# Picking one expert's rows in a TensorE loop over staged tiles, and one layer moved ahead of the transposes

## The chip, the core and the metric

The kernel runs on one core of a Trainium2 chip. A core has TensorE (matrix products, with its weight loads recorded apart), VectorE, ScalarE and GpSimd for the rest, and SyncE, which here only issues DMAs. One on-chip memory (SBUF) feeds all of them, and TensorE's results land in the eight banks of another (PSUM). The engines run side by side and wait for each other by counters (semaphores). The metric is the device time of one execution in microseconds (us), as the median of several.

## What is computed

Sparse attention over 4 batches x 8 heads x 576 positions, then a mixture of eight experts over the 2304 tokens, then one more feed-forward layer over all tokens. The change lies between the first and the second. This is the mixture:

```python
skip_score = x @ w_skip                  # x: 2304 tokens x 512
xc = x[skip_score > 0]
logits = xc @ w_gate                     # 8 experts
e_idx = argmax(logits); gate_w = softmax(logits)[e_idx]
for e in range(8):
    mask = e_idx == e
    h = relu(xc[mask] @ w1[e])           # 512 x 1024
    y[mask] = gate_w[mask] * (h @ w2[e]) # 1024 x 512
out[do_compute] = xc + y
```

## The kernel before, in words

The attention leaves x transposed in `XT` (512 rows of x as 4 blocks of 128 partitions, 2304 columns). The tokens must then be sorted by expert. The steps in order:

- TensorE turns each of the 18 tiles of 128 tokens back into rows (L967), ScalarE copies them into `xrow` (L572, counter `rows_copied`). VectorE meanwhile works out the expert and the place of every token and, for each tile t, a mask `hot(t)` of 128 x 168 that says which token goes to which of the first 168 sorted places (L736, counter `hot_ready`).
- GpSimd scatters each tile's rows to their sorted place in DRAM, `x_sorted` (L469, 18 indirect DMAs, counter `scattered`).
- TensorE doesn't wait for that round trip. It picks the first expert's 168 rows itself: for each of the four column blocks c it sums over the 18 tiles `xrow[:, t, c]` times `hot(t)` into bank `first_b[c]` (L995, unrolled; one float32 matmul of the code is two MATMUL and two LDWEIGHTS records, so 144 products). Each finished c raises `first_picked`; VectorE copies c = 0 and 2 (L765), ScalarE c = 1 and 3 (L580).
- `into(0)`: first layer of expert 0 (L1031, 64 products), ScalarE's `relus` (L588) behind it.
- `second_rows()`: the 168 rows of the second expert, loaded from `x_sorted` (SyncE L380 and L381, once `scattered` is full), are transposed (L1002) and copied by VectorE and ScalarE (L767, L592).
- `sort_turned()`: all sorted rows come back from DRAM into `xrow` by six loads (SyncE L385, which wait for `first_picked` to be 4, since they overwrite `xrow`), are transposed tile by tile (L1014, 72 transposes; L1018 for the gates) and copied into `XT` by VectorE (even tiles, L777) and ScalarE (odd tiles, L596), through the four banks `bank[2:6]`.
- `into(1)`, then `outof(0)`: second layer of expert 0 (L1041), whose results go to the same four banks. From expert 2 on, `into(e)` and `outof(e-1)` alternate.

Two side chains matter. The gates go through DRAM: VectorE copies them (L781), SyncE stores them (L396) and waits, and GpSimd, once they are stored and all of `XT` is sorted, copies the window of expert 2 (L476), which `into(2)` waits for. And SyncE issues its DMAs in the order of the code: the second expert's rows, the six loads, `w2` of expert 1 (L386), two small ones, then `w1` of expert 2 after `into(0)`.

Counters of TensorE's own products, such as `first_picked`, are raised when the product is done. All code of TensorE is unrolled here, apart from a loop over the attention's middle steps (L938), which runs three times, and one over the later groups of the last layer.

Of the kernel before, what the change touches and what calls it, by code (L numbers as in the profile page):

```python
# [9 lines left out]
F32 = mybir.dt.float32  # L10
# [8 lines left out]
P = 128  # L19
# [5 lines left out]
NT = N // P  # L25
# [88 lines left out]
def program(nc, qT, kT, vl, vs, wg, w1, w2, win, wout, cst, out):  # L114
    with ExitStack() as ctx:
        def sem(name):
            return ctx.enter_context(nc.semaphore(name))
# [37 lines left out]
        gateT, _, o = at("gateT", [GATES * E, NT // GATES, P], F32, p_at)  # L155
        gates, _, o = at("gates", [P, NT // GATES, GATES * E], F32, o)
        assert o <= r_end

# [97 lines left out]
        scattered, pads_out = sem("scattered"), sem("pads_out")  # L256
        gates_flat = sem("gates_flat")
        slots_in, hot_ready, first_picked, first_copied = sem("slots_in"), sem("hot_ready"), sem("first_picked"), sem("first_copied")
        second_in, second_turned, second_copied = sem("second_in"), sem("second_turned"), sem("second_copied")
# [24 lines left out]
        def hot(t):  # L284

            return XT[:, t % DC, WIN * (t // DC):WIN * (t // DC + 1)]
# [14 lines left out]
        def _(sp):  # L301
# [80 lines left out]

            sp.wait_ge(first_picked, DC)
            for g in range(NS):
# [148 lines left out]
        def _(act):  # L533
# [36 lines left out]
            for t in range(NT):  # L570
                act.wait_ge(rows_ready, t + 1)
                act.copy(xrow[:, t, 0:D], row_b[t % 4][:, :]).then_inc(rows_copied, 1)  # L572
                if t == EXP_AT:
                    act.wait_ge(dif_ready, 1)
                    act.activation(ex[:, :, :], dif[:, :, :], ACT.Exp).then_inc(exp_ready, 1)

            act.wait_ge(more_ready, 1)
            for c in range(1, DC, 2):
                act.wait_ge(first_picked, c + 1)
                act.copy(xw[:, 0, c, :], first_b[c][:, 0:WIN]).then_inc(first_copied, 1)  # L580
# [10 lines left out]
            act.wait_ge(second_turned, 2)  # L591
            act.copy(xw[:, 1, :, P:WIN], second_b[1][:, 0:DC * (WIN - P)].rearrange("p (c n) -> p c n", c=DC)).then_inc(second_copied, 1)  # L592

            for t in range(1, NT, 2):
                act.wait_ge(xt_ready, t + 1)
                act.copy(XT[:, :, P * t:P * (t + 1)], sort_b[t % 4][:, :].rearrange("p (c n) -> p c n", c=DC)).then_inc(xt_act, 1)  # L596
            more_n = act.value_load(n_more[0:1, 0:1], min_val=0, max_val=EXTRA)
            for e in range(1, E):
                relus(e, e % 2)
# [52 lines left out]
        def _(dve):  # L652
# [108 lines left out]


            for c in range(0, DC, 2):
                dve.wait_ge(first_picked, c + 1)
                dve.tensor_copy(xw[:, 0, c, :], first_b[c][:, 0:WIN]).then_inc(first_copied, 1)  # L765
# [85 lines left out]
        def _(pe):  # L851
# [137 lines left out]

            for c in range(DC):  # L990
                for t in range(NT):
                    if c == 0:
                        pe.wait_ge(rows_copied, t + 1)
                        pe.wait_ge(hot_ready, t + 1)
                    last = pe.matmul(first_b[c][:, 0:WIN], xrow[:, t, P * c:P * (c + 1)], hot(t), start=(t == 0), stop=(t == NT - 1))  # L995
                last.then_inc(first_picked, 1)

# [36 lines left out]
            def outof(e, par, loads):  # L1034
                pe.wait_ge(w2_in[par], 16 * loads)
                for c in range(DC):
                    behind(pe, y_scaled, DC * (e - 1) + c + 1)
                    for f in range(FEC):
                        if c == 0:
                            pe.wait_ge(h_done, FEC * e + f + 1)  # L1040
                        last = pe.matmul(y_b[c][:, 0:WIN], WE2[:, par, f, P * c:P * (c + 1)], hid[:, par, f, :], start=(f == 0), stop=(f == FEC - 1))  # L1041
                    last.then_inc(y_ready, 1)

            into(0, 0, 0, 1)
            second_rows()
            sort_turned()
            into(1, 1, 1, 1)

            pe.wait_ge(xt_dve, NT // 2)
            pe.wait_ge(xt_act, NT // 2)  # L1050
            outof(0, 0, 1)
# [139 lines left out]
```

## Time and profile before

| | us |
|---|---|
| median of 3 runs | 687.55 (687.15 to 689.2) |
| profiled execution | 690.49 |
| its span, first to last instruction | 688.4 |
| TensorE busy in it | 655.7 (95%) |
| picking (L995), first start to last end | 92.19 to 128.4 |

The span is the time between the first and the last instruction of one profiled execution; 2.1 us lie around it. Times inside it are counted from its start. Engines are named in the rows as PE (TensorE), PEld (its weight loads), DVE (VectorE), ACT (ScalarE), POOL (GpSimd) and SPq (SyncE's queue of DMA issues). A busy time says nothing by itself: an engine that waits for nobody and for whom nobody waits costs nothing. The chain of waits is what sets the end.

### The profile page before, as it was taken

Reading aid. Unit: us, or ns where it says so; the run is one execution under the profiler, and the core shown is the slowest. Engines: PE = TensorE matmul, PEld = TensorE weight load, DVE = VectorE, ACT = ScalarE, POOL = GpSimd, SP = SyncE. Lnnn points to the kernel's source line nnn. Section 1 sums busy time; section 2 is a strip of 40 time slices with the busy share of each in tenths; the row PEclk is TensorE's granted clock in tenths of the full one; section 3 lists DMA queues with packets and bytes.
Section 4 is the critical chain, followed back from the end, with each engine's and each line's share of the span. In section 5 each row is a group of like instructions: output and inputs, shape, how many; then the busy total and the mean of one; then the engine's idle time right before and its main releaser. Section 6 shows DMA issues by size and latency. Waiting matters only on the chain.

```text
span 688.4 us, 12667 instructions
## 1 busy us (share of the span) xinstructions
PE 655.7 (95%) x5265; PEld 567.6 (82%) x5266; DVE 317.6 (46%) x588; ACT 187.8 (27%) x361; POOL 126.1 (18%) x134
## 2 busy tenths in 40 slices
PE   7888995999999999999999999999999999999995
PEld 3776694999999999878888888888888888888994
DVE  4767460042121121676456544456444565545652
ACT  2455440141111111132224222232222332223331
POOL 1333155003222224882000200002000020000201
PEclk9999995999999999999999999999999999999999
DMA  8686595495777775230000100001000010000100
GB/s 279 207 282 206 181 388 186 172 357 160 259 256 261 263 274 189 85 115 17 0 1 1 61 1 0 1 0 61 0 0 0 0 61 0 0 0 1 62 0 31
DMA packets 39469, 76.09 MB, mean 111 GB/s; under 512 B 2967, under 2 KB 18012, under 8 KB 38916
## 3 DMA queue, kind: packets, MB, share of 16 engines
q1 hardware_dynamic: 36548, 66.00, 28.1%
q0 software_dynamic: 2880, 9.52, 3.6%
q8 instruction: 29, 0.48, 0.3%
q14 instruction: 12, 0.10, 0.0%
HBM read 65.57 MB, written 9.94 MB: 110 GB/s over the span
## 4 chain that ended last, share of the span: by engine, by line
PE 90%; DMA 4%; DVE 2%; issue 2%; SPq 1%; POOL 1%; ACT 0%; DVEq 0%
PE pair L1077 28%; PE pair L1096 16%; PE bank L1096 13%; PE pair L1031 11%; PE out_pair L1041 5%; PE bank L1041 5%; DMA k_loc<-kT 2%; PE pair L995 2%; PE out_pair L920 2%; PE pair L878 2%; PE out_pair L995 2%; DMA k_str<-kT 1%; PE bank L898 1%; PE bank L1014 1%; DVE yl L812 1%
## 5 line engine op out<-in xcount | busy, mean ns | idle before, releaser
L1077 PE MATMUL pair<-yh,WIH 128*128 128x512 f32 (+1 forms) x316 | 114.2, 368 | 0.2 <-ACT yh L609 0.2
L1077 PE MATMUL pair<-yh,WIL 128*128 128x512 f32 (+1 forms) x316 | 114.1, 368 | 0.0
L633 ACT ACTIVATE cl<-cl,half 128x512 f32<-128x512 f32 (+1 forms) x80 | 54.4, 680 | 185.1 <-DVE cl L833 183.7
L841 DVE TENSOR_TENSOR gl<-gr,gh 128x512 fp32r<-128x512 f32 (+1 forms) x80 | 54.5, 681 | 73.2 <-ACT gh L642 72.0
L833 DVE TENSOR_SCALAR cl<-pair 128x512 f32<-128x512 f32 (+1 forms) x79 | 50.3, 636 | 71.0 <-PE pair L1077 70.9
L528 POOL DMA_INDIRECT out<-XT,tok x18 | 18.6, 1031 | 349.4 <-DVE XT L821 345.4
L1077 PE MATMUL pair<-yl,WIH 128*128 128x512 f32 (+1 forms) x316 | 77.8, 368 | 0.4 <-DVE yl L812 0.4
L1031 PE MATMUL pair<-xw,WE 128*128 128x168 f32 x512 | 74.3, 306 | 0.5 <-ACT xw L580 0.5
L1031 PEld LDWEIGHTS pair<-xw,WE 128*128 128x128 f32 x512 | 73.3, 190 | 0.7 <-issue 0.7
L642 ACT CAST gh<-gr 128x512 fp32r<-128x512 f32 (+1 forms) x80 | 46.3, 579 | 85.6 <-PE bank L1096 58.3
L1077 PEld LDWEIGHTS pair<-yh,WIH 128*128 128x128 f32 x316 | 59.5, 188 | 11.0 <-ACT yh L609 0.6
L1077 PEld LDWEIGHTS pair<-yh,WIL 128*128 128x128 f32 x316 | 59.5, 188 | 10.3
L1077 PEld LDWEIGHTS pair<-yl,WIH 128*128 128x128 f32 x316 | 56.0, 189 | 10.6 <-DVE yl L812 0.8
L1096 PE MATMUL pair<-WOH,gh 128*128 128x512 f32 x160 | 62.6, 391 | 1.0 <-DVE gl L841 0.9
L839 DVE TENSOR_TENSOR gr<-gr,cl 128x512 f32<-128x512 f32 (+1 forms) x80 | 53.1, 664 | 21.9 <-ACT cl L633 21.6
L1096 PE MATMUL pair<-WOL,gh 128*128 128x512 f32 x160 | 62.4, 390 | 0.0
L1096 PE MATMUL pair<-WOH,gl 128*128 128x512 f32 x160 | 62.1, 389 | 0.0
L1096 PE MATMUL bank<-WOH,gh 128*128 128x512 f32 x128 | 49.8, 389 | 0.0
L1096 PE MATMUL bank<-WOL,gh 128*128 128x512 f32 x128 | 49.8, 389 | 0.0
L1096 PE MATMUL bank<-WOH,gl 128*128 128x512 f32 x128 | 49.8, 389 | 0.0
L836 DVE TENSOR_SCALAR gr<-pair 128x512 f32<-128x512 f32 (+1 forms) x79 | 49.5, 627 | 0.0
L588 ACT ACTIVATE hid<-pair 128x168 f32<-128x168 f32 x64 | 19.9, 311 | 108.3 <-PE pair L1031 108.3
(154 smaller groups left out, 849.6 us busy)
## 6 DMA issues: line engine op xcount, KB each, us to landing
WE<-w SPq DMA_DIRECT2D x16, 2048.0 KB, 10.9
xrow<-x_sorted SPq DMA_DIRECT2D x6, 781.5 KB, 9.8
v_loc<-vl SPq DMA_DIRECT2D x4, 1024.0 KB, 6.7
raw_in<-win SPq DMA_DIRECT2D x16, 256.0 KB, 9.2
raw_out<-wout SPq DMA_DIRECT2D x16, 256.0 KB, 2.6
q_loc<-qT SPq DMA_DIRECT2D x4, 576.0 KB, 5.3
k_loc<-kT SPq DMA_DIRECT2D x4, 576.0 KB, 6.9
v_str<-vs SPq DMA_DIRECT2D x8, 256.0 KB, 4.4
```

The costliest lines, as they stand in the source:

```text
L588: act.activation(hid[:, par, f, :], hid_b[f % 2][:, 0:WIN], ACT.Relu).then_inc(h_done, 1)
L633: act.activation(cl[:, 0:n], cl[:, 0:n], ACT.Square, bias=half[:, :], scale=0.5).then_inc(squared, 1)
L642: act.copy(gh[:, f % 2, 0:n], gr[:, 0:n]).then_inc(g_high, 1)
L833: dve.tensor_scalar(cl[:, 0:n], h2_of(g, f)[:, 0:n], -1.0, 1.0, ALU.max, ALU.min).then_inc(clamped, 1)
L836: dve.tensor_scalar(gr[:, 0:n], h2_of(g, f)[:, 0:n], 1.0, -1.0, ALU.max, ALU.add).then_inc(over, 1)
L839: dve.tensor_tensor(gr[:, 0:n], gr[:, 0:n], cl[:, 0:n], ALU.add).then_inc(g_ready, 1)
L841: dve.tensor_tensor(gl[:, f % 2, 0:n], gr[:, 0:n], gh[:, f % 2, 0:n].bitcast(F32), ALU.subtract).then_inc(g_low, 1)
L995: last = pe.matmul(first_b[c][:, 0:WIN], xrow[:, t, P * c:P * (c + 1)], hot(t), start=(t == 0), stop=(t == NT - 1))
L1031: last = pe.matmul(hid_b[f % 2][:, 0:WIN], WE1[:, par, c, P * f:P * (f + 1)], xw[:, buf, c, :], start=(c == 0), stop=(c == DC - 1))
L1041: last = pe.matmul(y_b[c][:, 0:WIN], WE2[:, par, f, P * c:P * (c + 1)], hid[:, par, f, :], start=(f == 0), stop=(f == FEC - 1))
L1077: last = pe.matmul(h2_of(g, f)[:, 0:tokens], w[:, c, P * f:P * (f + 1)], x[:, c, 0:tokens], start=(not low and c == 0 and k == 0), stop=(l ...
L1096: last = pe.matmul(fin_b[t][:, :], x[:, f % 2, P * t:P * (t + 1)], w[:, f, :], start=(f == 0 and k == 0), stop=(f == FFC - 1 and k == 2))
```

## The change

The picking now runs tile by tile: for each tile the four column blocks are multiplied one after the other into the four banks, which stay open over all tiles. Tile 0 and tile 17 are read from `xrow` as before. Tiles 1 to 16 are read from a new ring `stage` of four tiles, which ScalarE fills by copies from `xrow` after its last row copy, so that a TensorE loop of four passes over four tiles has fixed addresses for its weights. Two counters link the two: `staged` and `tile_picked`. `first_picked` is raised once, at the end. `into(1)` moves ahead of `sort_turned()` on TensorE, its `relus(1, 1)` ahead of the copies on ScalarE, and `outof(0)` waits for VectorE's copies ahead of its first and for ScalarE's ahead of its second column block.

```diff
+        stage, _, o = at("stage", [P, DC, D], F32, o)
...
-            sp.wait_ge(first_picked, DC)
+            sp.wait_ge(first_picked, 1)
...
+            for t in range(1, NT - 1):
+                behind(act, tile_picked, t - DC)
+                act.wait_ge(rows_copied, t + 1)
+                act.copy(stage[:, t % DC, :], xrow[:, t, 0:D]).then_inc(staged, 1)
+
             act.wait_ge(more_ready, 1)
+            act.wait_ge(first_picked, 1)
             for c in range(1, DC, 2):
-                act.wait_ge(first_picked, c + 1)
                 act.copy(xw[:, 0, c, :], first_b[c][:, 0:WIN]).then_inc(first_copied, 1)
...
+            relus(1, 1)
             for t in range(1, NT, 2):
                 act.wait_ge(xt_ready, t + 1)
...
-            for e in range(1, E):
+            for e in range(2, E):
                 relus(e, e % 2)
...
+            dve.wait_ge(first_picked, 1)
             for c in range(0, DC, 2):
-                dve.wait_ge(first_picked, c + 1)
...
-            for c in range(DC):
-                for t in range(NT):
-                    if c == 0:
-                        pe.wait_ge(rows_copied, t + 1)
-                        pe.wait_ge(hot_ready, t + 1)
-                    last = pe.matmul(first_b[c][:, 0:WIN], xrow[:, t, P * c:P * (c + 1)], hot(t), start=(t == 0), stop=(t == NT - 1))
-                last.then_inc(first_picked, 1)
+            def pick(rows_of_tile, table, first, last):
+                for c in range(DC):
+                    picked = pe.matmul(first_b[c][:, 0:WIN], rows_of_tile[:, P * c:P * (c + 1)], table, start=first, stop=last)
+                return picked
+
+            pe.wait_ge(rows_copied, 1)
+            pe.wait_ge(hot_ready, 1)
+            pick(xrow[:, 0, :], hot(0), True, False)
+            assert (NT - 2) % DC == 0
+            with pe.Fori(0, (NT - 2) // DC) as i:
+                for t in range(1, DC + 1):
+                    pe.wait_ge(staged, DC * i + t)
+                    pe.wait_ge(hot_ready, DC * i + t + 1)
+                    pick(stage[:, t % DC, :], XT[:, t % DC, bass.ds(WIN * i + WIN * (t // DC), WIN)], False, False).then_inc(tile_picked, 1)
+            pe.wait_ge(rows_copied, NT)
+            pe.wait_ge(hot_ready, NT)
+            pick(xrow[:, NT - 1, :], hot(NT - 1), False, True).then_inc(first_picked, 1)
...
                 for c in range(DC):
+                    if isinstance(e, int) and e == 0 and c < 2:
+
+                        pe.wait_ge(xt_act if c else xt_dve, NT // 2)
...
             into(0, 0, 0, 1)
             second_rows()
+            into(1, 1, 1, 1)
             sort_turned()
-            into(1, 1, 1, 1)
-
-            pe.wait_ge(xt_dve, NT // 2)
-            pe.wait_ge(xt_act, NT // 2)
             outof(0, 0, 1)
```

## Rows read from the trace of the kernel before

**Rows 1.** The page: TensorE's busy time, its 40 slices and its clock.

```profile
PE 655.7 (95%) x5265; PEld 567.6 (82%) x5266; DVE 317.6 (46%) x588; ACT 187.8 (27%) x361; POOL 126.1 (18%) x134
PE   7888995999999999999999999999999999999995
PEclk9999995999999999999999999999999999999999
```

**Rows 2.** Chain that ended last, in order of time: start us, us, what.

```profile
92.35 9.23 PE out_pair L995 x63
101.59 0.41 issue
...
106.23 0.28 PE pair L995
...
114.52 1.66 issue
...
117.62 10.78 PE pair L995 x58
...
128.86 9.36 PE pair L1031 x64
138.22 0.45 PE bank L1002 x4
...
147.74 9.12 PE pair L1031 x64
156.86 4.56 PE bank L1041 x32
...
165.98 9.12 PE pair L1031 x64
```

**Rows 3.** Busy us (and count) in stretches; clock, DMA share, GB/s; first three: L995 alone.

```profile
92.20:101.30 9.10, 9.10 (x63) 8.92 (x63) 1.00 1.03 396
102.00:117.60 15.60, 7.75 (x23) 5.36 (x23) 0.60 0.56 213
117.60:128.40 10.80, 10.77 (x58) 10.51 (x58) 0.79 0.11 32
...
120.00:124.00 4.00, 4.00 (x22) 4.00 (x22) 0.33 (x1) 0.00 (x0) 0.00 (x0) 0.72 0.00 0
...
136.00:140.00 4.00, 3.58 (x29) 3.30 (x28) 0.69 (x1) 1.20 (x4) 0.00 (x0) 1.00 1.05 391
```

**Rows 4.** DMA queues (packets, MB, share of 16), 98 to 100 us, then 102 to 117.

```profile
q0 software_dynamic: 136, 0.45, 57.1%
q1 hardware_dynamic: 94, 0.34, 41.5%
q8 instruction: 1, 0.02, 2.9%
...
q0 software_dynamic: 1004, 3.32, 57.8%
```

**Rows 5.** GpSimd's scatters; SyncE's issues (start us, us); what SyncE waited for.

```profile
L469 POOL DMA_INDIRECT x_sorted<-xrow,slot_of x18: 957/963/1142, 91.9 to 113.7; - x18
...
116.87 0.70 SPq L380 DMA_DIRECT2D xsecond<-x_sorted  x1
...
128.41 4.70 SPq L385 DMA_DIRECT2D xrow<-x_sorted  x6
...
SPq L385 <- PE pair L995: 10.4, 1, 10.4
```

**Rows 6.** Timeline of three engines: start us, us, what, [idle before <- releaser].

```profile
92.19 9.40 PE L995 MATMUL out_pair<-XT,xrow 128*128 128x168 f32 x63
...
90.80 4.01 DVE L736 TENSOR_SCALAR XT<-slots,posf 128x168 f32<-128x168 f32 x18
...
102.72 0.33 DVE L765 COPY xw<-out_pair 128x168 f32<-128x168 f32 x1 [4.58 <-remote]
...
92.28 1.25 ACT L572 COPY xrow<-pair 128x512 f32<-128x512 f32 x2
117.84 0.30 ACT L580 COPY xw<-out_pair 128x168 f32<-128x168 f32 x1 [24.31 <-remote]
```

**Rows 7.** The attention: chain at 34 to 37 us, TensorE's waits, queues 40 to 74.

```profile
34.64 0.37 PE bank L898 x2
35.01 1.82 issue
36.83 0.37 PE bank L898
...
PE bank L898 <- issue: 1.8, 1, 1.8
...
q1 hardware_dynamic: 4652, 8.11, 73.1%
q14 instruction: 2, 0.02, 0.1%
```

**Rows 8.** Output scatter: GpSimd's issues, and all engines' busy us in stretches.

```profile
552.65 0.96 POOL L528 DMA_INDIRECT out<-XT,tok  x1 [81.57 <-DVE XT L821]
...
552.00:556.00 4.00, 4.00 (x19) 3.30 (x18) 3.02 (x5) 0.81 (x3) 2.74 (x3) 1.00 0.32 122
556.00:560.00 4.00, 4.00 (x20) 3.30 (x19) 2.58 (x4) 1.81 (x3) 1.10 (x2) 1.00 0.37 140
```

**Rows 9.** ScalarE's copies, grouped: busy us, mean ns, idle before.

```profile
L642 ACT CAST gh<-gr 128x512 fp32r<-128x512 f32 (+1 forms) x80 | 46.3, 579 | 85.6 <-PE bank L1096 58.3 <-DVE gr L839 27.3
...
L572 ACT COPY xrow<-pair 128x512 f32<-128x512 f32 x10 | 5.9, 671 | 3.5 <-PE pair L967 3.5
```

**Rows 10.** Timeline around the end of the transposes: VectorE, TensorE, GpSimd.

```profile
139.44 1.09 PE L1014 MATMUL bank<-con,xrow 128*128 128x128 f32 x8 [0.42 <-DVE xw L767]
...
147.23 0.69 DVE L777 COPY XT<-bank 128x512 f32<-128x512 f32 x1
...
147.57 9.29 PE L1031 MATMUL pair<-xw,WE 128*128 128x168 f32 x64
...
155.24 0.74 POOL L476 COPY xw<-XT 128x672 f32 x1 [40.61 <-issue]
```

More of the change, by code:

```diff
@@ L257, in program @@
         gates_flat = sem("gates_flat")
+        staged, tile_picked = sem("staged"), sem("tile_picked")
         slots_in, hot_ready, first_picked, first_copied = sem("slots_in"), sem("hot_ready"), sem("first_picked"), sem("first_copied")
```

## The prediction

> **What bounds the kernel now.** I read five views, in this order: the page, the chain of waits in order of time, the idle time of TensorE's lines, the busy time by stretch, and the queues. The page says that TensorE is busy for 95% of the span, and that in the slices between 103 and 120 us its granted clock is half [rows 1]. So a gain has to come out of a place where TensorE stands still or runs at half clock. The chain has one such place, the picking of the first expert's rows (L995). Its 144 products start at 92.19 us [rows 6] and the last ends at 128.40 us [rows 2]. The first 63 start one every 0.144 us (9.10 us for 63). The next 23 take 15.6 us, and between them the chain shows "issue", which is time that no wait of the profile explains. The last 58 take 10.8 us, 0.186 us each [rows 2, 3]. At the pace of the first 63, all 144 would take 144 x 0.144 = 20.8 us. They take 36.2 us, so 15.4 us are lost: some 12.3 us in the 23 slow ones and some 2.4 us in the last 58, which start at the lower clock (0.79 in the mean of that stretch; the two levels are 1.2 and 2.4 GHz, and the fall comes after TensorE had stood still repeatedly). Behind the picking the chain is TensorE alone: the first layer of expert 0, the second expert's window, 72 transposes, the first layer of expert 1, the second layer of expert 0 [rows 2].
>
> What the stall is, is the whole question. Three things happen around it. One block of code (q8) is fetched between 98 and 100 us. GpSimd's 18 scatters of the rows run from 91.9 to 114.6 us, and their packets alone fill the queues from 102 to 117 us. SyncE, which waits for the scatters, goes on at 116.87 us, 0.75 us before TensorE is fluent again [rows 4, 5]. And the two engines that wait for TensorE's counter get it late: the first column block is finished at some 97.5 us, VectorE's copy of it starts at 102.72; the second at 106.2, ScalarE's copy starts at 117.84 [rows 2, 6].
>
> **The loop over staged tiles.** Two readings of the stall give two results. In the first, TensorE is short of code: a straight run of 144 products needs 288 instructions to be brought in while the queues are full, and a loop whose body is brought in once doesn't. For it: the attention's loop body runs three times, its only "issue" wait of TensorE (1.82 us) comes once, in the first pass, and in 34 us of the later passes the queues carry no packet of q8 [rows 7], whose packets of 16 KB come where TensorE's straight code goes on. Also for it: while the output is scattered by the same kind of DMA, four tiles at a time, TensorE stays busy 4.00 of 4 us [rows 8]. In the second reading the scatter itself slows whatever TensorE sends and receives. For that: the late counters above, and an end that falls on the scatter's end. I take the first, with little more than an even chance.
>
> The new picking then goes like this. Tile 0 is multiplied at once: 8 products x 0.144 = 1.16 us, to 93.35 us. ScalarE has its last row copy behind it at 93.53 us [rows 6]. It then copies tile 1 to the stage. That copy has no row of its own; the nearest are 579 ns (128x512 within the on-chip memory, L642) and 671 ns (the row copies L572, whose starts are 0.48 us apart) [rows 9]. I take 0.58 us: staged at 94.1 us, so TensorE waits 0.75 us. From there it needs 8 x 0.144 = 1.16 us for a tile and ScalarE at most 0.68 us, so ScalarE stays ahead, as long as the counter tile_picked, which frees a stage four tiles later, arrives in time (a rival, below). 17 tiles x 1.16 = 19.7 us, so the last product ends at about 114.0 us. The masks are no limit: VectorE has all 18 at 94.8 us [rows 6]. What the loop adds is two waits, a register or two and three jumps back. No row prices them; they lie in the queue ahead of the array, so between nothing and 1.8 us for each jump (the 1.82 us of [rows 7]); I take 0.5 us in all.
>
> The picks now end together, where before three of four columns were copied behind the next. So two copies on each engine stand on the path instead of one: +0.33 us [rows 6]. The first layer of expert 0 starts at 114.0 + 0.33 + 0.33 + 0.14 = 114.8 us instead of 128.86: 14.0 us earlier. What ScalarE gained to do (16 copies, 9.3 us) lies in 24.3 us in which it was idle [rows 6]. If that cover were gone, TensorE would wait for each tile.
>
> **What comes due next.** SyncE's order puts the second expert's window (L380) ahead of the sorted rows, and that waits for the scatters, to 116.87 us, whatever the picking does. Its own wait for the picking (10.4 us) goes [rows 5]. So the six loads of the sorted rows start at about 118 instead of 128.41 us. They are 4.7 MB and at the 390 GB/s of the stretch behind them [rows 3] take some 12 us, to 130 or 131 us. With the old order TensorE would want the first of them at 114.8 + 9.2 + 1.4 = 125.4 and the last some 7 us later, so they would cost up to 2 us there. With the first layer of expert 1 put before (9.1 us), the transposes start at 134.7 us and everything has landed. This is what the second part buys: not 9 us, but cover for 0 to 2 us. The window itself has landed by 120 us, when the queues are empty [rows 3], and is wanted at 124.
>
> **The second part by itself** moves 64 products ahead of 72 transposes on TensorE, and 8 activations ahead of 9 copies on ScalarE. VectorE's order stays. The wait for the window's copy (0.42 us, [rows 10]) only moves. The second layer of expert 0 now stands right behind the transposes and needs their last copies: VectorE's ends at 147.92 where TensorE is through at 147.57 [rows 10], so +0.4 us, which the first layer of expert 1 used to cover. GpSimd's window for expert 2 waits for all copies and for the gates' way through memory: 147.9 to 155.24, 7.3 us, with a weight load in the queues [rows 10]. It is wanted when the second layer of expert 0 ends: before the change at 165.98 us [rows 2], 18.3 us behind the transposes, after it 0.4 + 9.1 = 9.5 us behind them, with 7.3 + 0.74 us to go. It is hidden, but by 1.5 us only; if the gates came 2 us later it would show. I put it at nothing, because w1 of expert 2 follows the sorted rows in SyncE's order, and should be through by then.
>
> **Sum.** -14.0 + 0.4 + 0.5 = -13.1 us. The profiled execution took 690.49 us (span 688.4 and 2.1 around it), the median of the runs shown is 687.55, 2.9 us less. So 690.49 - 13.1 = 677.4 for a profiled execution and 674.5 us for the median, 1.9% less. All times below are medians.
>
> **Rivals.**
> (a) The loop pays for its jumps. If each of the three jumps back costs what the one code stall of the attention cost, 1.82 us [rows 7], 5.5 us of the gain go: 674.5 + 5.5 = 680 us. The Trainium skill has a rule that speaks for this (Runtime: NRT & Kernel Launch, Instruction fetch mechanics): prefetch is sequential, a taken branch whose target lies outside the buffered window must fetch first, hence its advice to unroll. The same section gives TensorE room for 2048 instructions. The passes without a fetched block in [rows 7] agree with the second sentence and speak against (a).
> (b) The stall belongs to the scatter, not to the code. Then TensorE is as far behind at 117.6 us as now, less 5 products for the 0.75 us wait: 63 instead of 58 are left, +0.9 us, and +0.33 and +0.4 us of the above. Nothing is gained: 687.55 + 1.6 = 689.2 us, within the measurement. For it: the late counters and the end of the stall. Against: [rows 8] and the single stall of [rows 7]. This is also the case in which the change doesn't do what it says.
> (c) Slower: the stage's ring closes on a late counter. A stage is free again when tile_picked reaches ScalarE, and between 97.5 and 117.6 us TensorE's counter was 5.2 and 11.6 us late [rows 2, 6]. The ring covers four tiles less a copy, 4 x 1.16 - 0.58 = 4.1 us. It decides from a lateness over 4.1 us. With 11.6 us, four tiles take 12.2 us: from tile 3 at 97.5 us it gets to tile 10 by 117.6 us, and with more instructions per tile in a throttled queue perhaps only to tile 6. Left are then 7 to 11 tiles x 8 x 0.186 = 10 to 16 us, against 10.8 now. With the 0.7 us above this is +0.5 to +6; I take +4: 691.5 us.
>
> **How the numbers follow.** Forecast 0.50 (its own range 673 to 678), (a) 0.07, (b) 0.23, (c) 0.20. A measurement of this kernel tells apart about 0.3%, 2 us, from no change. Faster by more than that: 0.57. Within: 0.22, which is (b) nearly whole. Slower: 0.21, which is (c) and the end of (b). Cases of both signs hold most of the chance, so the range reaches from the forecast's lower end to (b) and the first half of (c): 673 to 691.
>
> **What would show it.** In the changed kernel's profile: TensorE's "issue" between 98 and 118 us gone, and no half clock there; the last picking product at 114 us; ScalarE's stage copies 1.16 us apart after the fourth; the six sorted loads at 118 us; a wait of some 0.4 us ahead of the second layer of expert 0, and none for GpSimd's window behind it. For (b): "issue" gaps of the same kind inside the loop, ending near 117.6 us. For (c): TensorE waiting for ScalarE's stage copies, and these for TensorE, in rounds of four. For (a): a gap at every fourth tile. The prediction is wrong if TensorE is not through tile 12 by 110 us.

## The result, and the profile after

The changed kernel takes 691.3 us (median of 12), the kernel before beside it 687.4: a ratio of 1.0053 (95% interval 1.0031 to 1.0074), so 0.5% slower, where the prediction forecast 674.5 us in a range of 673 to 691. The profiled execution took 692.06 us (span 690.0), 1.6 us more than that of before.

The page of after, the lines that answer to [rows 1]. TensorE is busy for 2.6 us less than before in a span that is 1.6 us longer, so it stands idle for 4.2 us more, and the half clock stands in the same slice:

```profile
PE 653.1 (95%) x5266; PEld 566.0 (82%) x5266; DVE 318.3 (46%) x588; ACT 197.1 (29%) x377; POOL 125.9 (18%) x134
PEclk9999995999999999999999999999999999999999
```

The chain of waits of after, in order of time (start us, us, what), beside [rows 2]. The picking is L1001 now. "Another core or an unknown queue", and "remote" in the timelines, is a wait whose source the trace doesn't tell:

```profile
99.11 0.57 PE out_pair L1001 x4
99.68 1.08 PE pair L1001 x4
...
100.81 3.54 issue
104.35 0.02 ACT stage L583
104.37 9.07 another core or an unknown queue
...
113.49 2.86 another core or an unknown queue
...
116.38 0.63 ACT stage L583
...
117.23 1.48 PE out_pair L1001 x4
...
127.94 0.58 PE pair L1001 x4
128.52 0.02 issue
128.55 0.58 DVE xw L774 x2
...
129.26 9.36 PE pair L1050 x64
...
157.61 4.80 PE bank L1063 x32
```

Up to 100 us the loop runs as forecast, a tile every 1.14 us. Then 17 us pass in which the chain goes through ScalarE's stage copies and through something that it can't name. The first layer of expert 0 starts at 129.26 us, where it started at 128.86 [rows 2]. The picking itself began 1.14 us earlier than before (91.05 against 92.19 us), so from its first product on this is 1.5 us more.

The timeline of after, ScalarE and then TensorE (start us, us, what, [idle before <- releaser]):

```profile
92.09 2.33 ACT L583 COPY stage<-xrow 128x512 f32<-128x512 f32 x4
94.59 0.62 ACT L583 COPY stage<-xrow 128x512 f32<-128x512 f32 x1 [0.17 <-PE pair L1001]
96.52 0.62 ACT L583 COPY stage<-xrow 128x512 f32<-128x512 f32 x1 [1.31 <-PE pair L1001]
100.79 0.62 ACT L583 COPY stage<-xrow 128x512 f32<-128x512 f32 x1 [3.65 <-PE pair L1001]
104.35 0.62 ACT L583 COPY stage<-xrow 128x512 f32<-128x512 f32 x1 [2.95 <-issue]
113.47 0.62 ACT L583 COPY stage<-xrow 128x512 f32<-128x512 f32 x1 [8.50 <-remote]
116.38 2.18 ACT L583 COPY stage<-xrow 128x512 f32<-128x512 f32 x4 [2.29 <-remote]
...
101.64 0.83 PE L1001 MATMUL out_pair<-XT,stage 128*128 x4 [1.39 <-issue]
...
105.20 1.48 PE L1001 MATMUL out_pair<-XT,stage 128*128 x4 [2.16 <-issue]
...
114.34 1.48 PE L1001 MATMUL out_pair<-XT,stage 128*128 x4 [6.54 <-issue]
```

The copies of tiles 7, 8 and 9 start at 100.79, 104.35 and 113.47 us; TensorE takes these tiles up 0.85 to 0.87 us after each start. So TensorE waits for the stage (though two of its gaps are put down to "issue"), and ScalarE waits for `tile_picked`. Tile 9 may be copied when tile 5 is picked. TensorE was through with it at about 99 us, by the pace of 1.14 us a tile; the copy starts 14 us later. Tile 10 needs tile 6, which was picked at 100.25 us, and is copied at 116.38, 16 us later. The ring covers some 4 us of lateness. That is the wait that rival (c) names.

SyncE in after, beside [rows 5]. The loads of the sorted rows start where they did, since the picking ends where it did:

```profile
115.58 0.67 SPq L382 DMA_DIRECT2D xsecond<-x_sorted  x1
...
128.54 4.51 SPq L387 DMA_DIRECT2D xrow<-x_sorted  x6
```

### The profile page after: what moved, and what is told of

The parts are those of the page before. It is cut to its first block, busy times and chain, and to the rows that moved or that the text cites. A ratio compares the mean times of both kernels' runs of the same rounds, so it can differ in the third digit from the quotient of the medians.

```text
span 690.0 us, 12724 instructions
## 1 busy us (share of the span) xinstructions
PE 653.1 (95%) x5266; PEld 566.0 (82%) x5266; DVE 318.3 (46%) x588; ACT 197.1 (29%) x377; POOL 125.9 (18%) x134
## 4 chain that ended last, share of the span: by engine, by line
PE 85%; DMA 6%; DVE 2%; another core or an unknown queue 2%; ACT 2%; issue 1%; POOL 1%; SPq 1%; DVEq 0%
PE pair L1096 27%; PE pair L1115 16%; PE bank L1115 13%; PE pair L1050 10%; PE bank L1063 5%; PE out_pair L1063 5%; DMA k_loc<-kT 2%; DMA WE<-w 2%; PE out_pair L929 2%; PE pair L887 2%; PE out_pair L1001 1%; PE pair L1001 1%; ACT xrow L574 1%; DMA k_str<-kT 1%
## 5 line engine op out<-in xcount | busy, mean ns | idle before, releaser
L848 DVE TENSOR_TENSOR gr<-gr,cl 128x512 f32<-128x512 f32 (+1 forms) x80 | 53.0, 663 | 21.8 <-ACT cl L642 21.8
```

The source lines that it names most:

```text
L848: dve.tensor_tensor(gr[:, 0:n], gr[:, 0:n], cl[:, 0:n], ALU.add).then_inc(g_ready, 1)
```

## The experiments

The runs were made on five chips, here A to E. The kernel before took, as a median on each: A 688.7, B 676.7, C 689.2, D 676.6, E 690.1 us. That turned out to matter more than any edit. Every ratio is to the kernel before on the same chip. Each chip was used at one time only, so these runs can't tell the chip from the time.

**The scatter moved behind the picking (chip A).** Is the scatter the source? In both kernels GpSimd waits for the picking (for 1 instead of DC in the changed one):

```diff
+            pool.wait_ge(first_picked, DC)
             for t in range(NT):
                 pool.wait_ge(rows_copied, t + 1)
```

> The kernel before with one wait added: GpSimd begins its 18 scatters only when the picking is through (first_picked at 8). Nothing is left out. Scatter theory (the scatter delays what TensorE sends and receives): the picking takes 20.8 us (92.2 to 113.0 us), without 'issue' in the chain, at full clock, and both copies of the first two column blocks start within 0.1 us of their last product. Code theory (TensorE is short of instructions while queues are full): the queues are empty here too, so the picking is fluent as well, but with the counters of the column blocks as late as before only if something else delays them; so this run alone tells little between the two, and says only that the scatter is or isn't the source. If the stall belongs to neither (for example to the length of the straight code), it stays, at 98 to 118 us. The price: the scatters then run from 113 to about 136, SyncE's loads of the second window and the sorted rows behind them; the transposes, which ended at 147.6 us, end about 5 to 8 us later. Ratio to before expected 1.007 to 1.012. If the stall exists only in profiled executions, the timed runs would be worse by some 19 us instead (1.028).

> The changed kernel with the same wait: GpSimd begins its scatters when the picking is through (first_picked at 1). Nothing is left out. With the scatter out of the way the loop stands alone: if tile_picked is late only because of the scatter, the stage copies follow each other by 1.16 us, TensorE never waits for ScalarE over 0.1 us after the first tile, the picking takes 20.8 us plus 0.75 us (first stage) plus at most 0.5 us for the loop: 22 us, ending at 114.2 us. If the loop itself is slow (jumps back, a ring that is too short in any case), it takes 25 us or more, with gaps at every fourth tile. Against the kernel before with the same wait: the same or up to 1.5 us slower from the loop, and the second expert's first layer (9.36 us) now covers part of the wait for the sorted rows, so in the whole some 6 to 9 us faster than it; ratio to the kernel before 0.995 to 1.003.

Measured: 1.0168 (1.0125 to 1.0210) and 1.0132 (1.0083 to 1.0181). Timelines of the first (TensorE, ScalarE), then of the second (ScalarE):

```profile
88.91 10.43 PE L996 MATMUL out_pair<-XT,xrow 128*128 128x168 f32 x72
99.17 10.42 PE L996 MATMUL pair<-XT,xrow 128*128 128x168 f32 x72
...
99.42 0.30 ACT L581 COPY xw<-out_pair 128x168 f32<-128x168 f32 x1 [9.18 <-PE out_pair L996]
119.14 0.31 ACT L589 ACTIVATE hid<-pair 128x168 f32<-128x168 f32 x1 [1.64 <-PE pair L1032]
122.00 0.31 ACT L589 ACTIVATE hid<-pair 128x168 f32<-128x168 f32 x1 [2.55 <-remote]
```

```profile
94.06 0.62 ACT L584 COPY stage<-xrow 128x512 f32<-128x512 f32 x1 [0.52 <-PE pair L1002]
95.20 0.62 ACT L584 COPY stage<-xrow 128x512 f32<-128x512 f32 x1 [0.52 <-PE pair L1002]
```

Without the scatter beside it the unrolled picking has no gap (20.7 us), its counters are in time, and the ring never closes: the stage copies are 1.14 us apart. From the first product to the last, start to start, the loop takes 21.4 us and the unrolled form 20.4. The hold-up has moved with the scatters, which run from 110.62 us: of ScalarE's activations, 1.14 us apart until 117.19, the last two come 0.8 and 2.5 us late (119.14 and 122.00), while TensorE's products are fluent to their end at 119.43. So the scatter is needed for the stall, and the loop costs 1.1 us where nothing disturbs it. The price of the later scatter was underestimated in both (11.6 us instead of 5 to 8, and 9.1 instead of at most 2): the second expert's rows come late, and TensorE stands still for 18.9 us ahead of them in the trace of scatter_after.

**The two parts, one at a time.** `loop_only` is the first part alone. `layer_only` is the second alone, this swap with its waits and ScalarE's order:

```diff
-            sort_turned()
-            into(1, 1, 1, 1)
+            into(1, 1, 1, 1)
+            sort_turned()
```

> The changed kernel with the old order behind the picking: the sorted rows' transposes ahead of the first layer of expert 1, and both waits for the copies ahead of the second layer of expert 0. Nothing is left out. If the loop's ring alone makes the change slower, the whole difference is here: ratio 1.003 to 1.007, and the second layer of expert 0 starts as late as in the changed kernel or up to 0.5 us earlier. If the order costs too (copies of the last tiles, ScalarE's 8 activations ahead of its copies), this run is at 1.000 to 1.003.

> The kernel before with the second part of the change alone: the first layer of expert 1 ahead of the sorted rows' transposes, its activations ahead of ScalarE's last copies, the second layer of expert 0 waiting for the copies. Nothing is left out. By the forecast the order alone costs 0.4 us (the copies of the last tiles stand on the path); the sorted rows are loaded in time in either order. Ratio 1.000 to 1.001. If the order is what makes the change slower, 1.002 or more, and a new wait shows behind the transposes or at the gates.

Measured: the loop alone on A 1.0038 (1.0010 to 1.0067). The order alone on B 0.9953 (0.9932 to 0.9974). The second was a surprise, and its trace a greater one. TensorE and GpSimd on chip B:

```profile
91.68 10.43 PE L996 MATMUL out_pair<-XT,xrow 128*128 128x168 f32 x72
101.94 10.42 PE L996 MATMUL pair<-XT,xrow 128*128 128x168 f32 x72
...
91.39 1.14 POOL L469 DMA_INDIRECT x_sorted<-xrow,slot_of  x1 [17.22 <-ACT xrow L572]
...
113.15 0.96 POOL L469 DMA_INDIRECT x_sorted<-xrow,slot_of  x1 [0.30 <-issue]
```

The scatters run as in [rows 5], 18 of them over the same 22 us, the code of the picking is that of before, and there is no stall at all.

**The chip or the code?** The kernel before, the changed kernel and the second part were run again on other chips:

> The kernel before, unchanged, for its trace on this chip. The run of layer_only had a picking without any stall, while its text up to the end of the picking is that of the kernel before, and the kernel before took 676.7 us beside it, 12 us less than in the earlier call. If the stall belongs to the chip, the trace goes with the time: at some 688 us with 'issue' between 101 and 117 us and 36 us of picking, at some 677 us without, and 20.5 us of picking. If it belongs to the text of the kernel (layer_only shifts it), the stall is here at either time.

> The changed kernel, unchanged, timed on this chip. Where TensorE has no stall, the counter tile_picked is in time, ring and loop cost 0.75 us for the first stage, 0.33 us for the second copy and at most 0.5 us for the loop, and the order of the first layer of expert 1 gives back what it gave in layer_only (0.47% or 3.2 us with its interval from 0.26 to 0.68%): ratio 0.995 to 1.000. Where TensorE has the stall, as before: 1.003 to 1.007, with stage copies that follow late counters. A ratio over 1.002 without the stall would mean that the loop costs by itself.

> The kernel before with the first layer of expert 1 ahead of the transposes, once more. Nothing is left out. If the stall is absent on this chip, the ratio is 0.993 to 0.998 as before, since the sorted rows are loaded from 115 us on and the old order would want them at 123. If the stall is there, the sorted rows come late in either order (their loads start when the picking ends, and have 10 us to land): 0.999 to 1.002.

> The changed kernel once more, for the case that this chip has no stall, where it hasn't been timed yet: then the picking takes 21.5 to 22.5 us, the stage copies follow each other by 1.14 us, and the ratio is 0.995 to 1.000 (the order of the first layer of expert 1 gives 0.3 to 0.6%, the loop takes up to 0.2%). With the stall it is 1.003 to 1.007 again.

> The changed kernel with the old order behind the picking, once more. Nothing is left out. Without the stall: the changed kernel was at 0.9998 and the order of the first layer alone at 0.9953, so the loop should cost 0.2 to 0.6% by itself (of which the first stage and the second copy explain 1.1 us, 0.16%): 1.002 to 1.006. If the order and the loop don't add up so (the order gives nothing behind a shorter way), 1.000 to 1.001. With the stall: 1.001 to 1.007 as before.

| | chips with the stall | chips without it |
|---|---|---|
| kernel before, us | A 688.7, C 689.2, E 690.1 | B 676.7, D 676.6 |
| picking, first to last product, unrolled | 34.2 to 35.9 us (4 traces, without small_ops2) | 20.4 us (B) |
| the same, in the loop | 36.8 to 39.2 us (4 traces) | 21.4 us (D) |
| changed kernel | first measurement 1.0053, C 1.0053 (1.0022 to 1.0084) | D 0.9998 (0.9981 to 1.0015) |
| loop alone | A 1.0038, E 1.0035 (1.0010 to 1.0061) | not run |
| order alone | C 0.9990 (0.9959 to 1.0021) | B 0.9953 (0.9932 to 0.9974) |

The second and third lines are starts of the first and last picking product in the timelines. The stall goes with the chip, not with the code: `layer_again` on C is the kernel of `layer_only` on B, and has a stall of 15 us. The 12 us between the chips' medians fit the stall, less what it hides, but there is no trace of the kernel before itself on B, D or E; on D its executions spread from 675.2 to 685.3 us, so a stall in some of them isn't excluded. On a chip without it the changed kernel does what the prediction describes, in its timings too, and gains nothing. Chain of the changed kernel on chip D:

```profile
91.40 0.83 PE out_pair L1001 x4
...
110.47 0.58 PE pair L1001 x4
...
111.80 9.36 PE pair L1050 x64
...
122.42 9.36 PE pair L1050 x64
```

No gap stands at any of the loop's jumps back.

**Aligned rows (chip A).** `ROW` of 528 instead of 521 numbers:

> The kernel before with rows of 528 instead of 521 numbers in the row tile and in its copy in memory (2112 bytes, a multiple of 64, instead of 2084), the seven further columns set to zero. Nothing is left out. If the scatter stalls TensorE because its rows of 2084 bytes are cut at uneven places, the stall shrinks: the picking ends before 125 us instead of 128.4, ratio under 0.995. If it is the software-issued transfers as such, nothing changes: stall from 101 to 117 us, ratio 0.998 to 1.002.

Measured 0.9979 (0.9958 to 0.9999). The picking ends at 127.1 us, not before 125, with its stall from some 102 to 117.5 us. So the alignment isn't the cause; the ratio lies just under the 0.998 that was expected for this, and a gain of up to 0.4% from it isn't excluded.

**GpSimd's transfers or their bytes?** The 18 scatters become 18 plain stores by SyncE, the same tiles to the same buffer; the sorting is left out.

```diff
-                pool.indirect_dma_start(xs, bass.IndirectOffsetOnAxis(slot_of[:, t:t + 1], 0), xrow[:, t, :], None).then_inc(scattered, 16)
+                sp.dma_start(xs[P * t:P * (t + 1)], xrow[:, t, :]).then_inc(scattered, 16)
```

> The kernel before with the 18 scatters by GpSimd replaced by 18 plain stores of the same row tiles by SyncE, in the order of the tokens, to the same place in memory. The sorting of the rows is left out, so the experts get other rows; everything else stays. If the stall comes from transfers whose addresses GpSimd issues, it is gone: the picking takes 20.8 to 22 us and ends at about 113 to 114 us, with both first counters in time. If it comes from the bytes (3.8 MB out of the row tiles while TensorE reads them), the stall stays, some 10 to 15 us, wherever the stores run.

> As plain_store2, for a chip on which the kernel before takes some 688 us (the sorting of the rows is left out, the same rows go to memory in the order of the tokens by plain stores of SyncE). Stall from GpSimd's transfers: none here, picking 20.5 us. Stall from the bytes or the row tiles: 'issue' in the picking while the stores run. Where the kernel before takes some 677 us it tells nothing new.

Two runs fell on B and D and say nothing (674.2 and 671.6 us, picking fluent). The third fell on E, where the kernel before takes 690 us: 673.8 us. TensorE's timeline there:

```profile
91.36 10.43 PE L996 MATMUL out_pair<-XT,xrow 128*128 128x168 f32 x72
101.62 10.42 PE L996 MATMUL pair<-XT,xrow 128*128 128x168 f32 x72
...
129.44 1.09 PE L1015 MATMUL bank<-con,xrow 128*128 128x128 f32 x8 [0.57 <-DMA xrow<-x_sorted]
```

The queues are fuller than with the scatter (a DMA share of 1.06 from 102 to 110 us, against 0.56 in before_again), the bytes are the same, and there is no stall. So neither the bytes nor the reading of the row tiles is enough: it takes the scatters that GpSimd issues. Two things differ at once here, who issues the transfers and whether each row has an address of its own. Which of the two matters was not tested.

**Who is held up (chip C)?** VectorE and ScalarE get 150 and 60 copies of two columns, which need nothing and signal nothing:

```diff
+            for k in range(150):
+                dve.tensor_copy(tiny[:, k, :], con[:, C_ID:C_ID + 2])
```

> The kernel before with 150 copies of two columns on VectorE and 60 on ScalarE added ahead of their waits for the picking, so that both engines work while the scatter runs. Nothing is left out. If TensorE has its stall on this chip, two cases: the scatter holds up every engine that has many short instructions, and their starts spread between 101 and 117 us; or it holds up TensorE alone, and the copies follow each other at an even pace right through (60 to 200 ns each). Without the stall the run only says that the copies cost nothing.

Measured 690.4 us in one execution. VectorE's timeline, then the busy time by stretches (us, then PE, PEld, DVE, ACT, POOL with their counts, clock, DMA share, GB/s) of this kernel and of the kernel before on the same chip:

```profile
97.25 1.79 DVE L765 COPY tiny<-con 128x2 f32<-128x2 f32 x23
...
107.18 0.17 DVE L765 COPY tiny<-con 128x2 f32<-128x2 f32 x1 [1.22 <-issue]
107.89 0.17 DVE L765 COPY tiny<-con 128x2 f32<-128x2 f32 x1 [0.55 <-issue]
108.59 0.17 DVE L765 COPY tiny<-con 128x2 f32<-128x2 f32 x1 [0.53 <-issue]
...
116.29 7.28 DVE L765 COPY tiny<-con 128x2 f32<-128x2 f32 x103 [0.54 <-issue]
```

```profile
101.00:116.00 15.00, 3.89 (x10) 2.31 (x9) 3.19 (x20) 3.11 (x19) 9.60 (x10) 0.56 0.57 218
```

```profile
92.00:98.00 6.00, 6.00 (x44) 6.00 (x43) 4.26 (x19) 0.15 (x1) 4.78 (x5) 1.00 1.03 408
101.00:116.00 15.00, 7.05 (x24) 5.00 (x23) 0.00 (x0) 0.00 (x0) 9.47 (x10) 0.65 0.54 209
```

The copies come 0.08 us apart until 99 us, then one to three every 0.7 or 1.4 us, then again 0.07 us apart. TensorE, VectorE and ScalarE are held up together, and they share what is left: TensorE's two kinds of instructions fall from 47 to 19 in these 15 us, and VectorE and ScalarE get 39; together 58 against 47, where 107 were recorded in 6 us before the stall. GpSimd isn't held up: 18 scatters start over 21.8 us with the stall and without it (before, layer_only). It isn't TensorE's instruction supply, since copies on two other engines are held up at the same time, and it isn't signals alone, since these copies raise no counter. Nor is code fetched at any rate that would fit a start every 0.7 us. The queue of code from 92 to 117 us in before_again:

```profile
q8 instruction: 1, 0.02, 0.2%
```

**Does it take a run of scatters?** `layer_only`, with GpSimd waiting ahead of its seventh scatter:

```diff
+                if t == 6:
+                    pool.wait_ge(first_picked, DC // 2)
```

> layer_only with GpSimd's scatters in two parts: the first six at once, the other twelve when half of the picking is done (first_picked at 4/2, at some 102 us). Nothing is left out. On a chip with the stall it began some 8 to 9 us after the first scatter in every trace, about seven scatters later. If it needs such a run of scatters, it now begins at 110 us or later and TensorE has all but the last 15 instructions of the picking behind it: the picking ends before 116 us, and what stalls is the first layer of expert 0, until the scatters end at some 120 us; ratio 0.990 to 0.997. If it needs only some number of scatters since the start, it begins after the first one or two of the second part, ends at 120 us instead of 117, ratio 1.000 to 1.005. Without the stall: the second window lands 2.5 us later, ratio 0.995 to 1.000.

> layer_only with the first six scatters at once and the other twelve behind the picking (first_picked at 4). Nothing is left out. On a chip with the stall: the picking has none and ends at 113 us; the scatters end at 128.5, the second expert's rows are there at 132, TensorE waits for them from 122.5 us; the sorted rows land by 144, the transposes end at 150 to 152 instead of 156.9 us: ratio 0.991 to 0.996. If six scatters are enough to start the stall, it shows from 101 to some 103 us and the gain is 1 to 2 us less. Without the stall it is worse than layer_only by some 10 us: ratio 1.008 to 1.012.

> As split_mid (first six scatters at once, twelve behind half of the picking, the first layer of expert 1 ahead of the transposes), for a chip with the stall: if the stall needs a run of some seven scatters, TensorE is fluent to 109 us or later and the ratio is 0.990 to 0.997; if it counts scatters since the start, it begins at 103 to 104 us and the ratio is 1.000 to 1.005. Without the stall, 0.994 to 0.999 again.

Measured: split_mid on D 0.9965 (0.9936 to 0.9994), on E 0.9917 (0.9882 to 0.9951), where the stall is. split_end on D 1.0160 (1.0143 to 1.0177), some 3 us above the upper end of what was expected: in its trace the chain runs through the twelve later scatters and the second expert's load, and TensorE gets to that window only at 135.6 us. Timelines of split_mid2 on E: GpSimd, TensorE, ScalarE, VectorE:

```profile
96.94 0.96 POOL L471 DMA_INDIRECT x_sorted<-xrow,slot_of  x1 [0.30 <-issue]
101.44 0.96 POOL L471 DMA_INDIRECT x_sorted<-xrow,slot_of  x1 [3.54 <-PE out_pair L998]
...
101.00 10.42 PE L998 MATMUL pair<-XT,xrow 128*128 128x168 f32 x72
119.14 11.35 PE L1034 MATMUL pair<-xw,WE 128*128 128x168 f32 x64 [7.71 <-ACT xw L582]
...
118.70 0.30 ACT L582 COPY xw<-pair 128x168 f32<-128x168 f32 x1 [17.14 <-remote]
...
99.13 0.33 DVE L768 COPY xw<-out_pair 128x168 f32<-128x168 f32 x1 [2.53 <-remote]
```

The picking has no gap to its end at 111.4 us, though six scatters have run before 98 us and eight more by 111. Two of its four counters are late. The last product ends at 111.43, and ScalarE's copy starts at 118.70. And the first six scatters aren't without effect: the first column block ends at 95.94 us, and VectorE, idle for 2.53 us, copies it at 99.13, 3.2 us later. The first layer of expert 0 starts at 119.14, against 125.7 (C) and 128.9 us [rows 2]. So a pause of 3.5 us puts TensorE's first gap off by 10 us (111.4 against 101.3 us in before_again on C, whose picking starts at 90.8 us, as here at 90.6). The pause wasn't run without the second part.

**Wider products (chip B).** The mask as the weight and rows of 512 columns moving, 36 products instead of 72:

> The kernel before with the operands of the picking exchanged: the mask is the weight (40 or 128 slots), the row tile of 512 columns is what moves, so 36 products of 512 columns instead of 144 of 168; then 8 transposes bring the picked rows into the old layout. Nothing is left out. At 0.144 us for 168 columns a product of 512 should take 0.44 us, 36 of them 15.8 us. If the scatter holds up TensorE by instruction (some 0.7 us for a load and a product, whatever their size), the 36 products hardly feel it: the last ends at about 108 to 110 us, but its counter reaches VectorE only when the scatter is through (some 117 us), and the first layer of expert 0 begins at about 120 instead of 128.9 us: 8 to 9 us earlier, ratio 0.986 to 0.990. If it holds TensorE up by time (it stands still for 15 us, whatever it has to do), the last product ends at about 123 to 125 us, the first layer begins at 126 to 128, ratio 0.995 to 1.000.

Measured 1.0138 (1.0112 to 1.0164). My expectation priced a product by one record; it has two, as the text above says of those of 168 columns. They took 72 x 0.434 = 31.2 us instead of 20.5, which is more than the loss of 9.3 us. On this chip there was no stall to be seen through, so the question that it was made for stayed open there.

## Why the prediction was wrong

**What the stall is** is the step that failed: the reading that TensorE is short of code there, so that a loop ends the stall, and with it the term of -14.0 us. Measured, the first layer of expert 0 started 0.4 us later, not 14.0 us earlier. I took the code reading "with little more than an even chance". It is refuted: with the same code and the same scatters there is no stall on B; with GpSimd's transfers replaced there is none on E; and on C VectorE and ScalarE stall as well. What the runs showed in its place is a hold-up that comes with GpSimd's run of scatters and makes counters up to 16 us late. What I took for evidence was none:
- [rows 8] was put against the scatter, since TensorE stays busy in the output scatter. Those are four transfers at a time. In split_mid2 six in a row make one counter 3.2 us late and stop no product; TensorE's first gap in the unrolled picking came 9 to 11 us after the first of an unbroken run. A load that comes in small portions says nothing of a long run.
- [rows 7] and the block of q8 showed that code can stall TensorE once, not that it did here.
- The late counters were the right sign, and they stood in the rows: a shortage of code on TensorE doesn't explain the lateness of a counter whose product is done. They also came first: the first column block was finished at 97.48 us, 4 us before TensorE's first gap.

**Rival (c)** is what happened, with 0.20 as its chance: a ring of 4 us against counters that were 4 us late at tile 7 and 14 at tile 9. It forecast tile 10 at 117.6 us (117.23 in the trace) and 691.5 us (691.3 measured). The wait is the one that it names; that its numbers fit is luck in part. It had four tiles take 12.2 us from 97.5 us on; in the trace the pace was full to tile 6, and tiles 7 to 9 then took 17 us. And its +4 us was 3.3 us for the ring, where the picking took 1.3 us longer in the two traces of the result (37.16 against 35.89 us), and 0.7 us for copies. With +0.28, +0.51 and +0.6 us from the next paragraphs the traces show 2.7 us from the first picking product on, within the measured +3.9 (2.1 to 5.1). The forecast named as its refutation that TensorE wouldn't be through tile 12 by 110 us; it was through tile 8.

**The loop's own price** was right in kind. Forecast 0.75 for the first stage and 0.5 us for the loop; start to start, 21.44 against 20.38 us where nothing disturbs it, 1.1 us. Rival (a) and the Trainium skill's rule on taken branches (Runtime: NRT & Kernel Launch, Instruction fetch mechanics) find no support: all four passes follow each other without a gap on D. They say nothing against the rule for a target outside its window, which no run here has been shown to have. With the stall the loop takes 1 to 5 us more than the unrolled form (36.8 to 39.2 against 34.2 to 35.9, some of them on different chips); in `after` its tiles 7 to 10 wait for late counters, which straight code doesn't.

**The copies together, and the copies behind the transposes**: forecast +0.33 and +0.4 us. From the last picking product to the first of the second layer of expert 0 the traces have 28.62 (before), 28.90 (loop alone), 29.13 (order alone) and 29.41 us (both): +0.28 and +0.51.

**What the second part buys** was forecast as cover for 0 to 2 us if the picking ends early. Where it does, it gave 3.2 us (1.8 to 4.6) on B; the 0.57 us in the row of plain_store3 is one of the waits that it covers. The rest of the 3.2 us isn't explained, since there is no trace of the kernel before on B. Where the picking ends late, it gave nothing that can be measured (C).

**What wasn't in the sum**: in all traces of the loop the last layer starts 0.6 to 1.0 us later behind the first product of `outof(0)` than without it (128.2 to 128.5 against 127.6 us). Of it, a weight load that lands 0.3 to 0.7 us late is seen; the rest isn't explained. On D and B the two parts then add up to about what was measured: -3.2 for the order, +1.1, +0.3 and some 0.7 for the loop, against -0.1 (-1.3 to +1.0).

So of the terms of the sum the small ones were sound, and the one large one, the stall's end, was not to be had: where there is a stall the loop doesn't end it, and on the others it isn't there.

## What to carry to other kernels

When an engine stalls without a wait, look whether its counters arrive late and whether other engines stall too, before its code is blamed; a few tiny instructions on idle engines show it, here at no cost that one execution shows (690.4 us; the kernel before took 685.7 to 695.1 on that chip). Don't put a ring that lives on prompt counters into such a stretch; straight code with few handshakes lost 1 to 5 us less. Try to break a long run of scatters issued by GpSimd by a pause that costs nothing: six, then twelve behind half of the picking, together with the second part of the change, was faster than the kernel before on a chip with the stall (0.8%) and on one without it (0.35%). On the latter the second part alone would explain the gain (0.9953 on B); on the former it gave nothing alone (0.9990 on C), which speaks for the pause. And before a gain of 2% is forecast from a stall, see whether it is there on another chip.

## What the runs showed of the hardware

The same kernel takes 677 us on two chips and 689 on three. What the traces show between them is one hold-up of TensorE, VectorE and ScalarE, 15 us long, while GpSimd issues 18 scatters in a row: these engines start some 3 to 4 instructions per us in all, where 18 were recorded before. The scatters themselves keep their pace. The first counter that is late was raised 5 to 8 us after the first scatter (at 97.48 and 91.89 us in the kernel before, at some 118 and 110.62 in scatter_after), and TensorE's first gap in the unrolled picking comes 9 to 11 us after it (9.7 in the kernel before). The hold-up ends some 4 us after the last scatter's start and delays counters by up to 16 us (tile 10 in after). TensorE's granted clock is 0.65 in the mean of these 15 us and falls to the lower level (1.2 GHz), after TensorE has stood still repeatedly.

What the engines share there is not settled. A buffer for something that each instruction sends, filled faster than it is drained, would fit the late start, the pause that puts it off, the common budget and the late counters; why GpSimd keeps its pace would still have to be explained. The Trainium skill has such a thing (NOTIFIC — the notification-queue block, The census, and Overflow: three behaviours, one of which stalls the engine): the records of all engines of a core go through one unit, and its internal queues hold the engines back rather than lose a record. By that, the stall could be a price of being recorded. No run here shows it or tests it: all executions that were timed have a recorded span and clock, and the 12 us between the chips are in all of them. Nor is it known why two chips have none.
